# First three attention chunks prepared side by side, and the gate's column work moved into the prologue

## The reference

```python
# attention: q, k, v, a_re, a_im are (4, 8, 768, 48)
mag = np.sqrt(a_re * a_re + a_im * a_im)
scale = np.minimum(mag, 0.999) / (mag + 1e-06)
...
for t in range(S):
    new_re = ar * S_re - ai * S_im
    new_im = ar * S_im + ai * S_re
    S_re, S_im = (new_re + kv, new_im)          # kv = outer(k_t, v_t)
    y[:, :, t] = np.einsum('bhd,bhde->bhe', q[:, :, t], S_re)
...
# MLP on x of (3072, 384), d_ff 2048
h = x @ w_in
g = h * np.tanh(log1p(exp(h)))
x2 = g @ w_out
# mixture of experts
logits = x2 @ w_gate + modality_bias[modality_id]
e_idx = np.argmax(logits, axis=1)
out[token] = gate_w * (relu(x2 @ w1[e]) @ w2[e])
```

## Time and profile before

| | us |
|---|---|
| median of 3 runs | 1104.81 (1103.52 to 1107.12) |
| profiled execution | 1103.16 |
| its span from first to last instruction | 1101.4 |
| PE busy in the span | 980.2 (89%) |
| DVE, ACT, POOL busy | 712.3, 625.5, 80.6 |

### The profile page before, as it was taken

One profiled execution on the slowest core, in us unless ns is written; L12 is line 12 of the kernel. 1 busy time (PEld: TensorE's weight loads), 2 busy tenths in 40 slices (PEclk: granted clock), 3 DMA queues, 4 the chain that ended last, 5 costly groups with the idle time before them and its releaser, 6 DMA issues.

```text
span 1101.4 us, 19052 instructions
## 1 busy us (share of the span) xinstructions
PE 980.2 (89%) x6516; PEld 946.6 (86%) x6517; DVE 712.3 (65%) x1288; ACT 625.5 (57%) x1185; POOL 80.6 (7%) x138
## 2 busy tenths in 40 slices
PE   2557989999999999999999999995279999879996
PEld 0446889899999999999999999994269999879996
DVE  4363479898888897888897876775533333463332
ACT  5353668687677787677777765561034444444442
POOL 1000000000000000000000000000012222322222
PEclk9985889999999999999999999997669999999999
DMA  6521011112112122122121110000151111331110
GB/s 179 152 51 36 16 23 37 37 37 58 37 37 58 37 51 57 33 43 58 38 58 37 22 44 8 1 22 24 65 194 36 43 36 43 137 134 43 41 38 29
DMA packets 146164, 58.66 MB, mean 53 GB/s; under 512 B 131257, under 2 KB 140487, under 8 KB 146096
## 3 DMA queue, kind: packets, MB, share of 16 engines
q1 hardware_dynamic: 139280, 42.63, 16.0%
q0 software_dynamic: 3616, 10.43, 3.0%
q10 hardware_dynamic: 3200, 4.72, 1.2%
HBM read 48.21 MB, written 10.03 MB: 53 GB/s over the span
## 4 chain that ended last, share of the span: by engine, by line
PE 84%; DVE 6%; issue 3%; ACT 2%; DMA 2%; SPq 1%; ACTq 0%; POOL 0%; POOLq 0%; DVEq 0%
PE bank L1342 19%; PE bank L1323 18%; PE bank L1491 13%; PE bank L1502 10%; PE bank L1295 4%; PE bank L1263 3%; PE bank L1297 3%; PE bank L1271 3%; PE bank L1281 3%; PE bank L1249 1%; PE bank L1243 1%; PE bank L1358 1%; PE bank L1312 1%; PE bank L1474 1%; SPq L414 1%
## 5 line engine op out<-in xcount | busy, mean ns | idle before, releaser
L1491 PE MATMUL bank<-xg_t,w_sb 128*128 128x128 f32 x1296 | 157.4, 283 | 18.3 <-ACT he L784 16.9
L1491 PEld LDWEIGHTS bank<-xg_t,w_sb 128*128 128x128 f32 x1296 | 155.8, 199 | 19.5 <-ACT he L784 17.8
L1323 PE MATMUL bank<-x_hi,w_in_hi 128*128 128x384 f32 x384 | 142.3, 370 | 5.6 <-DVE w_in_lo L927 5.6
L1342 PE MATMUL bank<-w_out_hi,g_hi 128*128 128x392 f32 x384 | 141.1, 367 | 0.0
L1323 PE MATMUL bank<-x_lo,w_in_hi 128*128 128x384 f32 x384 | 131.6, 343 | 0.0
L1323 PE MATMUL bank<-x_hi,w_in_lo 128*128 128x384 f32 x384 | 131.5, 343 | 0.0
L1342 PE MATMUL bank<-w_out_hi,g_lo 128*128 128x392 f32 x384 | 130.6, 340 | 0.0
L1342 PE MATMUL bank<-w_out_lo,g_hi 128*128 128x392 f32 x384 | 130.5, 340 | 0.0
L627 ACT ACTIVATE hid<-bank 128x384 f32<-128x384 f32 x128 | 62.4, 488 | 90.7 <-PE bank L1323 89.8
L784 ACT ACTIVATE he<-bank 128x128 f32<-128x128 f32 x216 | 59.5, 277 | 65.9 <-PE bank L1491 59.5
L1212 DVE TENSOR_SCALAR he_m<-he 128x256 int32<-128x256 int32 x108 | 31.8, 294 | 78.8 <-ACT he L784 78.8
(11 more groups left out here) (208 smaller groups left out, 2106.8 us busy)
## 6 DMA issues: line engine op xcount, KB each, us to landing
w_sb<-in_moe_w_dram SPq DMA_DIRECT2D x8, 1536.0 KB, 7.2
ab<-in_a_re_dram SPq DMA_DIRECT2D x24, 192.0 KB, 2.9
ab<-in_a_im_dram SPq DMA_DIRECT2D x24, 192.0 KB, 3.1
qk_raw<-in_q_dram SPq DMA_DIRECT2D x24, 192.0 KB, 3.1
qk_raw<-in_k_dram SPq DMA_DIRECT2D x24, 192.0 KB, 3.3
v_in<-in_v_dram SPq DMA_DIRECT2D x24, 192.0 KB, 2.7
x_rows<-x_sb ACTq DMA_DIRECT2D x8, 576.0 KB, 3.0
w_in_sb<-in_moe_w_in_dram SPq DMA_DIRECT2D x4, 768.0 KB, 8.7
```

Source lines behind the costliest of these rows:

```text
L1323: last = mm(bank_h[f % 2][:, 0:TT], w[:, kk, f * P:(f + 1) * P], x[:, m % 2, kk], start=(kk == 0 and i == 0), stop=(kk == KD - 1 and i == 2))
L1342: last = mm(bank_x2[t][:, 0:DE], g[:, u % RING, f % QF, t * P:(t + 1) * P], w[:, f], start=(f == 0 and i == 0), stop=(f == FT - 1 and i == 2))
L1491: last = mm(bank_h[f % 2][:, 0:P], w1_sb[par][:, kk, f * P:(f + 1) * P], xg_t[:, kk], start=(kk == 0), stop=(kk == KD - 1))
```

## The change

The prologue is written anew on every engine, and three further things go with it.

- Chunks 1 and 2 get buffers of their own for the prologue (`sq_first`, `mag_first`, `seed_first`, `frac_first`, `cs_first`, `ee_first`, `qk_hat_first` and others), chunk 4 gets one for its angle, and sums, turns and transposes are spread over more PSUM banks. The magnitudes of chunks 0 to 2 are made first, then one load of the Sin and Arctan table serves the Arctan and the waves of all three, then one load of the other table follows. Chunks 3 and 4 are begun in the prologue too: the Arctan of both and the waves of chunk 3 take one more pair of loads.
- The angle sums of chunks 1 and 2 no longer wait for a carried row. PE adds the whole sum of the earlier chunks with a matrix of equal entries (`all_turns`): one, two and three products for chunks 0, 1 and 2.
- The row copies of chunks 0 to 3 (`gl`) and the carried rows into chunks 3 and 4 are issued on POOL's queue. SP issues `w_out` in four pieces near the start, then `w_in`, and `mod_raw` and `bias_rows` after the loads for chunks 3 to 5.
- Of the gate's 16 steps, 9 turns and copies stand in the prologue, one behind each piece of attention work, and the other 7 in slot 0, one for each gap from 0 on. The gate's columns are taken at gap 8 in place of 9.

```diff
-    GATE_FROM, GATE_TO = 1, 1 + WL
+    GATE_FIRST, GATE_TO = 9, 8
...
             decays_load(0)
             decays_load(1)
+            sp.dma_start(wg_sb[:], w_gate.rearrange("(k p) e -> p k e", p=P)).then_inc(wg_in, 16)
+            w_out_load(0)
+            decays_load(2)
             qk_load(0)
...
+            for x in range(FIRST):
+                first_row(x)
+            first_carry(FIRST - 1)
+            first_row(FIRST)
+            first_carry(FIRST)
...
+            def first_row(x):
+                pool.wait_ge(ee_ready, 2 * x + 1)
...
+                for twice in range(2):
+                    pool.dma_start(of(x, gl, gl_first)[:, twice],
+                                   heads(of(x, ee, ee_first)[C - 1:C, 0])).then_inc(gl_first_in[x], 16)
...
+            def first_carry(x):
+                pool.wait_ge(frac_ready, x + 1)
+                pool.wait_ge(hat_ready, 2 * FIRST)
+                pool.dma_start(carry_of(x + 1), of(x, frac, frac_first)[C - 1:C, 0]).then_inc(carry_first_in[x + 1 - FIRST], 16)
...
+            def first_turns(x):
+                pe.wait_ge(angle_ready, x + 1)
...
+                last = mm(turn_bank(x)[:, 0:DM], turn_sum[:], angle_of(x), start=True, stop=(x == 0))
+                for y in range(x):
+                    last = mm(turn_bank(x)[:, 0:DM], all_turns[:], angle_of(y), start=False, stop=(y == x - 1))
+                last.then_inc(turns_summed, 1)
...
+            def gate_step(k):
+                if k > 0:
+                    gate_product(k - 1)
+                if k < FT:
+                    gate_turn(k)
...
-                    if m == 0:
-                        if GATE_FROM <= g < GATE_TO:
-                            gate_turn(2 * (g - GATE_FROM))
-                            gate_turn(2 * (g - GATE_FROM) + 1)
...
+                    if m == 0 and g <= FT - GATE_FIRST:
+                        gate_step(GATE_FIRST + g)
```

More of the change, by code:

```diff
@@ L416, in _ @@
                          ).then_inc(small_in, 16)
-            for ch in range(NCH):
+            for ch in range(FIRST, NCH):
                 if ch + 1 < NCH:
@@ L843, in logs @@
                                          ).then_inc(logs_ready, 1)
             def fractions(x):
[L846 removed]
+                turns, f = turn_bank(x)[:, 0:DM], of(x, frac, frac_first)
                 dve.wait_ge(turns_summed, x + 1)
[L848 to L850 removed]
+                wait(dve, cs_ready, 2 * before(x))
@@ L1064, in _ @@
             straight(dve.memset(state[:], 0.0))
[L1065 to L1068 removed]
+            for x in range(FIRST):
+                mags(x)
+                slopes(x)
+                logs(x)
             fractions(0)
[L1070 to L1072 removed]
+            fractions(1)
+            dve.wait_ge(zero_out, 16)
             hats(0)
[L1074 to L1085 removed]
+            fractions(2)
+            hats(1)
+            decay_columns(0)
+            hats(2)
+            mask(0, 0)
+            mask(0, 1)
+            take_kv(0)
+            next_state(0)
+            decay_columns(1)
+            mags(3)
+            slopes(3)
+            logs(3)
+            mask(1, 0)
+            mask(1, 1)
+            take_kv(1)
+            next_state(1)
+            decay_columns(2)
+            mags(4)
+            slopes(4)
+            mask(2, 0)
+            mask(2, 1)
+            take_kv(2)
+            next_state(2)
+            logs(4)
+            add_carry(3)
+            attend(0, 9)
+            attend(1, 9)
+            split_w_in(0)
+            attend(2, 9)
+            fractions(3)
+            add_carry(4)
+            hats(3)
             for m in range(NT):
@@ L1439, in slow_mlp @@
                     last.then_inc(s_x2_ready, 1)
-            sums(0)
-            for ch in range(CT):
-                for p in range(10):
-                    attend(ch, p)
+            first_logs(0)
+            gate_step(0)
+            first_logs(1)
+            gate_step(1)
+            first_logs(2)
+            gate_step(2)
+            first_turns(0)
+            first_turns(1)
+            first_turns(2)
+            gate_step(3)
+            gate_step(4)
+            decay_columns(0)
+            turn_qk(0, 0)
+            turn_qk(0, 1)
+            turn_qk(0, 2)
+            turn_qk(0, 3)
+            gate_step(5)
+            turn_qk(1, 0)
+            scores(0, 0)
+            turn_qk(1, 1)
+            scores(0, 1)
+            turn_qk(1, 2)
+            key_values(0)
+            turn_qk(1, 3)
+            decay_columns(1)
+            outputs(0, 0)
+            outputs(0, 1)
+            gate_step(6)
+            turn_qk(2, 0)
+            scores(1, 0)
+            turn_qk(2, 1)
+            scores(1, 1)
+            turn_qk(2, 2)
+            key_values(1)
+            turn_qk(2, 3)
+            decay_columns(2)
+            outputs(1, 0)
+            outputs(1, 1)
+            gate_step(7)
+            scores(2, 0)
+            scores(2, 1)
+            key_values(2)
+            turn_y(0)
+            outputs(2, 0)
+            outputs(2, 1)
+            turn_y(1)
+            gate_step(8)
+            turn_y(2)
+            fourth_logs()
+            fourth_turns()
             for m in range(NT):
```

467 lines of the change are left out of this document (308 added, 159 removed).

## The result

The changed kernel took 1068.62 us (median of 4 runs, 1063.63 to 1071.9) against 1104.16 (4 runs, 1097.51 to 1107.12) beside it: a ratio of 0.9682, 95% interval 0.9623 to 0.9741. The forecast was 1068, in a range of 1060 to 1083. The profiled execution took 1067.44, its span is 1065.7. By those the forecast stands some 3 us too high.

The account below looks back on a forecast made before the run. Before slot 1, chunks wait on a chain across engines, with no engine full in the prologue. Slot 0 starting at 70 plus 98.6 gives 168.6 against 204.85, 36.2 us less: 1067.0 profiled, 1068 forecast, range 1060 to 1083.

Parts of the forecast that it names:

- Magnitudes and angles: Prologue, first stage: third magnitude done near 16.9 us, angle sums done at 25 to 29, first turned block copied near 34.
- The clock in the prologue: Prologue: low clock until about 35 us and a second short fall around 30, giving slot 0's start at 70.
- The list of PE's work at the full clock: Rest of the prologue: PE's work sums to 32.2 us, putting slot 0's start at 67.3 at the full clock throughout.
- T1: Start of slot 0, PE's first product of hidden(0, 0): forecast at 70 us, against 103.82 in the kernel before.
- The carried row: Prologue: DVE's 10.73 us wait for the row, copied by SP behind `mod_raw` and `bias_rows`, would go.
- Slot 0: Length of slot 0: 101.0 less 9.9 for nine gate steps plus 7.5 of new PE wait, 98.6 us.
- SP's small loads: Slot 0: `mod_raw` and `bias_rows` hold SP's queue for 10.8 us again, covered by a us or so, costing nothing.
- rival 4: Slot 0: SP's two small loads delay the row carried from chunk 4; chance 0.02 slower than before, 0.02 milder (1081 us).
- The sum: Whole kernel: slot 1 begins 36.2 us earlier, so the profiled execution falls from 1103.16 to 1067.0 us; forecast 1068.
- T2: Start of slot 1, PE's first product of hidden(1, 0): forecast at 168.6 us, against 204.85 in the kernel before.
- Rival 2: Prologue and slot 0: full clock comes early and stays, POOL's carried row lands as fast as SP's; 1062 us, chance 0.13.
- Rival 3: Slot 0: each of POOL's three transfers waits for a DVE instruction of 1.75 us, 5.3 in all; 1073 us, chance 0.08.

Follow-up runs that it names:

- a_wide_fill: The changed kernel plus five unused wide products in PE's idle time of 3.36 us in the prologue: slot 0 begins at 66.97 us against 70.20.
- b_small_last: The kernel before, with the loads of `mod_raw` and `bias_rows` moved to the end of SP's loop: slot 0 begins at 97.88 us against 103.82.
- b_wout_late: The kernel before, with the gate's weights, `w_out` and the small loads behind the carried row and last row into chunk 1: slot 0 begins at 99.97 us.
- a_gate_back: The changed kernel with all 16 gate steps back in slot 0: slot 0 begins at 66.11 us and takes 105.58, slot 1 begins at 171.69.
- a_hidden_ahead: The changed kernel, with PE running hidden(0, 1) and a gate step ahead of the sums of chunk 4: slot 0 takes 94.30 us against 94.19.
- a_small_last: The changed kernel with `mod_raw` and `bias_rows` at the end of SP's loop: slot 0 begins at 69.68 us and takes 94.20.
- a_whole_sum4: The changed kernel with chunk 3's sum added by `all_turns` in place of the carried row into chunk 4: slot 0 takes 91.27 us against 94.19.
- c_best: The changed kernel with earlier ACT copies of chunk 0, chunk 3's sum by `all_turns`, and an earlier first `w_in` split: 1058.76 us, ratio 0.9590 to before.
- a_again: The changed kernel once more, unaltered: 1064.75 us against 1103.86 for the kernel before.
- a_table_pairs: The changed kernel with two more pairs of table loads in the prologue: slot 0 begins at 71.08 us against 70.20 and takes 99.12 against 94.19.

## Why the prediction was right, and where its steps were off

1. *Magnitudes and angles.* Right: the third magnitude's logarithm done at 17.22 (16.9), the angle products begun at 21.71 (21.3) and ended at 27.5 (25 to 29), the first copy at 34.05 (34). The order of the queues and the durations of before were enough. One sign was missed without harm: four table loads lie before slot 0, not five, and the fifth is at 72.67.

2. *The clock in the prologue.* "I take the low clock until about 35, and a second short fall in the sparse stretch around 30" was wrong in its place. It was full from 25 to 32 already, and low once, from 32 to 42.3, behind PE's wait of 3.36 for the first copy. The price was right, partly by luck: 2.7 us by the prediction (70 less 67.3), 3.2 by a_wide_fill. The list of PE's work at the full clock gave 67.3; with that clock it took 66.97. So T1 came out at 70.20 for 70. The list has seven of the nine gate steps; the other two ran from 27.4 to 30.3, where PE had to wait for the first copy anyway.

3. *The carried row.* The prediction, and with it the recorded text of b_small_last, calls the late row the one that chunk 1's angle needs. It is the one from chunk 1 into chunk 2. The row into chunk 1 left SP in the kernel before at 20.92, ahead of `w_out`, and DVE waited only 1.90 us for it:

```profile
20.92 0.66 SPq L367 DMA_DIRECT2D sq<-frac  x1
...
22.73 0.55 DVE L837 SCALAR_TENSOR_TENSOR angle<-sq,angle 1x384 f32<-1x384 f32 x1 [1.90 <-DMA sq<-frac]
```

The late row held up chunk 0 as well, since DVE's masks of chunk 0 stand behind `add_carry` in its queue: PE waited 8.03 us for the masks. The prediction let the 10.73 us of waiting go because "the row copies are made early", and put them down to SP, held by `mod_raw` and `bias_rows`. That cause was read too simply. With SP freed the row leaves 8.5 us earlier and arrives 8.1 us after its issue while `w_out` is on the DMA engines (b_small_last); with `w_out` behind it, it lands after 1.7 (b_wout_late). Two things hold it, SP's queue and `w_out` on its way, and taking away one brings out the other. Neither edit gave more than 5.9 us of T1, and 3.7 of those are the clock's. What frees the changed kernel is that no early work of chunk 1 or 2 needs a copied row for its angle at all.

4. *The rest of the 33.6 us* is overlap and the clock. PE's idle time of the prologue fell by 32.5 us, but part of that is filled with the gate's steps. With the gate's steps out of both prologues (a_gate_back against before) T1 is 37.7 us less: 25.6 us of idle time, and 12.1 of busy time with no less work, which is the clock's. How much of the idle time is due to side by side buffers alone was not measured. The one table load for all is a small part: two more pairs cost T1 0.9 us at most.

5. *Slot 0.* 98.6 was predicted, 94.19 measured; this is the term that was mis-sized. PE's idle time in the slot rose by 4.0 us (7.0 to 11.0) where the sum has 7.5, and its busy time fell by 10.9 (94.0 to 83.2) where the sum has 9.9. The wait at the sums is 4.94 us, since the last copy is used 1.5 us after its issue and not 3.4, and POOL's issues take 0.50 and not 0.72. The work of the nine gate steps was sized rightly, 9.8 us of busy time (a_gate_back); the other 1.1 us of busy time has the clock's mark, 0.90 in slot 0 before and 0.93 now, which the sum left out. In the prologue the four steps on the path were to cost 4.4 us, and 4.1 were measured. That is partly luck: nine steps added 11.0 us of busy time there, and without them the low stretch from 32.7 on is also 3.4 us shorter. As for the length of the wait, a_hidden_ahead filled it and the slot was no shorter, because the clock took back what the filling had brought.

6. *SP's small loads.* Covered, as predicted, and shorter than in before: 3.2 us and not 10.8. a_small_last has slot 0 at 94.20 with or without them, so rival 4 had nothing to stand on.

7. *The sum.* T2 came out 4.2 us lower than predicted (164.39 for 168.6), the rest of the profiled execution 4.7 us longer, at least 3.2 of them by chance, and so its time of 1067.44 met 1067.0. That the two numbers agree so closely is luck: two misses of opposite sign. With the usual rest the kernel takes 1064 to 1065. Rival 2 (1062) stood nearer with its slot 0 of 96.4 than the forecast did.

8. *Rival 3, POOL's copies behind DVE.* The copies of POOL landed after 1.5 to 5.6 us:

```profile
L600 POOL DMA_DIRECT2D cs_first<-frac_first x1: 502/502/502, 37.3 to 37.3; - x1
...
DMA to landing us min/median/max: 1.5/3.3/5.1
```

The one at 37.3 took 5.1 us with DVE nearly idle (0.69 us busy of 5.1) and the DMA engines full (a share of 1.02); the one at 75.75 took 1.5 with the engines empty (0.02) and DVE idle too. So the landing goes with the load of the DMA engines here, though not by it alone: copies of `ee` issued under full engines landed after 2.6 us (issued at 19.73) to 5.6 us (at 12.60). The ones at 12.60 had DVE busy for 4.1 of 5.4 us beside them, and landed 5.2 and 5.6 us after their issue, hardly later than the one with DVE idle. Whether DVE's copies can delay POOL's issues, as the Trainium skill says in "SBUF — State Buffer", section "SBUF: two separate sides", is not told apart by this, and the three copies of slot 0 have no DVE work beside them. The Trainium skill's page "DMA: Bandwidth & Descriptors", section "Queues, rings and completion order", says that a DMA engine takes its queues in turn. The traces don't contradict it: under full engines the row on POOL's own queue landed in 5.1 us, the one on SP's, behind `w_out`, in 8.1.

**What stays open.** Why the clock falls at slot 0's wait in one kernel and not in another. a_whole_sum4 and c_best have the same order and nearly the same wait there (2.92 and 3.24 us); in the one it stays full, in the other it falls. a_hidden_ahead has only 1.64 us of waiting and it falls. In the front of the program the fall is repeated (a_again has the same T1 and T2), but behind the expert's wait of 3.59 us the clock is full in a_again and was low in the first execution of the same program. On what it depends isn't shown. What it costs was seen: about 2.6 us for a fall in slot 0, 3.2 in the prologue, each some 10 us long, and 4.6 us of busy time where it lasted 10 us longer (a_table_pairs). Open too is whether SP's own queue or the full DMA engines hold the carried row once SP is free: no run puts that row on a queue of its own with `w_out` under way.

## What to carry to other kernels

Where chunks wait for a chain over several engines, count the idle time of the matrix engine and ask how much of its work could stand side by side: here, with the gate's steps left out, 25.6 of 37.7 us were idle time. The other 12.1 came with it, as PE ran more of its work at the full clock. A small copy that another engine waits for has to be kept out of stretches with large loads, by queue and by time, or made unneeded by a product more. After filling a wait, look at idle and busy time apart: the idle time can fall as planned and the gain go to a lower clock.

## What the runs showed of the hardware

- Work without a use can shorten a kernel: five wide products (3.4 us) in a wait of 3.36 us kept the granted clock at full for the 10 us behind it and brought 3.2 us. In slot 0 the same trick moved the fall to the next wait, made it shorter and brought 0.7 us.
- A copy of 1.5 KB took 1.5 to 1.7 us to land with the DMA engines nearly idle, and 2.6 to 8.1 us with them full, the 8.1 on SP's queue behind 3 MB of `w_out`.
- The issue of a finely cut load depends on what is queued ahead: `bias_rows` held SP for 8.35 and 8.49 us behind 3 MB of `w_out`, and for 2.33 with little queued.
- The front of the program repeats to 0.1 us from one execution to the next, while the part from slot 7 on takes 411.8 or 415.0 us with the same instructions, by the clock that it is granted behind two waits of 3.59 and 3.21 us.
